# Joining the block inverses of a delta-rule layer to 64x64: two solves and one carry for each step in place of four and three

## The reference, cut to what matters

```
k_n = k / (norm(k) + 1e-6)
for t in range(768):
    y[t]  = q[t] @ state
    state = state + beta[t] * outer(k_n[t], v[t] - k_n[t] @ state)
```

## Time and profile before

| | us |
|---|---|
| median of three runs | 834.78 |
| profiled execution, its own time | 835.71 |
| its span | 834.0 |
| PE busy | 793.1 (95%) |
| DVE busy | 569.0 (68%) |
| ACT busy | 369.1 (44%) |
| POOL busy | 112.6 (14%) |

### The profile page before, as it was taken

One profiled execution on the slowest core, in us unless ns is written; L12 is line 12 of the kernel. 1 busy time (PEld: TensorE's weight loads), 2 busy tenths in 40 slices (PEclk: granted clock), 3 DMA queues, 4 the chain that ended last, 5 costly groups with the idle time before them and its releaser, 6 DMA issues.

```text
span 834.0 us, 29247 instructions
## 1 busy us (share of the span) xinstructions
PE 793.1 (95%) x12158; PEld 724.2 (87%) x12159; DVE 569.0 (68%) x1504; ACT 369.1 (44%) x1042; POOL 112.6 (14%) x281
## 2 busy tenths in 40 slices
PE   5978999999999999999999999999999989999994
PEld 3557888899989999889999999999999989999993
DVE  6967887878578685777777677654323667767751
ACT  3722443434435353443434535343543556666641
POOL 1000000001010010101002010000103054344441
PEclk9989999999999999999999999999999999999998
DMA  8743112121211223112220211211023546655610
GB/s 271 219 160 123 46 53 66 60 89 48 92 48 40 91 65 97 42 50 87 66 91 22 66 47 66 64 41 47 32 86 118 186 133 208 198 191 184 188 32 14
DMA packets 46649, 79.75 MB, mean 96 GB/s; under 512 B 5680, under 2 KB 35082, under 8 KB 46144
## 3 DMA queue, kind: packets, MB, share of 16 engines
q1 hardware_dynamic: 43104, 73.07, 27.1%
q0 software_dynamic: 3424, 4.93, 1.9%
HBM read 67.05 MB, written 13.19 MB: 96 GB/s over the span
## 4 chain that ended last, share of the span: by engine, by line
issue 79%; POOL 9%; DMA 6%; POOLq 2%; PE 2%; DVE 1%; ACT 0%; SPq 0%
DMA id_table<-token,slot 5%; POOL idle L680 3%; POOL kq_t L735 2%; POOL id_table L725 2%; PE psum L980 1%; POOL ids_all L731 1%; DMA id_table<-x_sb 1%; POOL out L790 1%; DMA kd<-kq 1%; POOLq L509 0%; POOLq L510 0%; PE psum L836 0%; POOLq L757 0%; POOL token L718 0%; PE psum L981 0%
## 5 line engine op out<-in xcount | busy, mean ns | idle before, releaser
L1014 PE MATMUL psum<-xt_hi,w_hi 128*128 128x256 f32 x768 | 226.3, 295 | 5.3 <-issue 2.7
L1015 PE MATMUL psum<-xt_lo,w_hi 128*128 128x256 f32 x768 | 217.5, 283 | 0.0
L1016 PE MATMUL psum<-xt_hi,w_lo 128*128 128x256 f32 x768 | 217.2, 283 | 0.0
L1190 ACT ACTIVATE h_raw<-psum 128x256 f32<-128x256 f32 x192 | 73.6, 384 | 311.0 <-PE psum L1016 309.3
L1449 DVE TENSOR_TENSOR h_lo<-h_raw,h_hi 128x256 fp32r<-128x256 f32 x192 | 81.4, 424 | 160.2 <-ACT h_hi L1191 159.4
L1014 PEld LDWEIGHTS psum<-xt_hi,w_hi 128*128 128x128 f32 x768 | 145.3, 189 | 14.5 <-issue 8.8
L1016 PEld LDWEIGHTS psum<-xt_hi,w_lo 128*128 128x128 f32 x768 | 146.3, 190 | 0.0
L1015 PEld LDWEIGHTS psum<-xt_lo,w_hi 128*128 128x128 f32 x768 | 145.8, 190 | 0.0
L1038 PE MATMUL psum<-w_hi,h_hi 128*128 128x394 f32 x384 | 138.6, 361 | 1.1 <-DVE h_lo L1449 1.1
L1040 PE MATMUL psum<-w_hi,h_lo 128*128 128x394 f32 x384 | 131.2, 342 | 0.0
L1039 PE MATMUL psum<-w_lo,h_hi 128*128 128x394 f32 x384 | 131.0, 341 | 0.0
(11 more groups left out here) (183 smaller groups left out, 1121.8 us busy)
## 6 DMA issues: line engine op xcount, KB each, us to landing
kq_t<-kq SPq DMA_DIRECT2D x24, 512.0 KB, 3.6
bp<-moe_w SPq DMA_DIRECT2D x24, 512.0 KB, 4.5
kv_t<-kv SPq DMA_DIRECT2D x24, 384.0 KB, 3.1
bp<-moe_w SPq DMA_DIRECT2D x24, 384.0 KB, 4.2
kd<-kq SPq DMA_DIRECT2D x20, 256.0 KB, 3.3
x_table<-x_sb SPq DMA_DIRECT2D x13, 392.0 KB, 2.8
out<-x_sb SPq DMA_DIRECT2D x12, 384.0 KB, 3.1
bp<-moe_w_in SPq DMA_DIRECT2D x6, 512.0 KB, 6.0
```

The costliest lines, as they stand in the source:

```text
L1014: m(out, hi, x_hi, start=first, stop=False)
L1015: m(out, hi, x_lo, start=False, stop=False)
L1016: return m(out, lo, x_hi, start=False, stop=last)
L1190: a_.activation(h_raw[i % 2][:, :], up_ps[i % 2][:, 0:G2], ACT.Silu)
```

## The change

**Joining inverses.** After the 32x32 inverses of a quad are ready, they are transposed a second time (`turn_first`, DVE). For each head and each pair of neighbouring blocks (0,1) and (2,3), PE multiplies the key block between them with the first block's inverse (`met`, 16 products of 32x32 by 32 columns for a step), ACT copies the result (`keep_met`), PE multiplies it with the second inverse (`grow`, 16 more), and DVE puts the product beside the two inverses (`grow`, two operations on 128 x 128 elements for a step), where ACT has spread them (`halves`, two copies of 128 x 512 for a pair). The result, `grown`, holds the inverses of 64x64 blocks. It lies in the old tiles `inv` and `dg`.

**The chain.** A step now has solve 0, carry, solve 1. A solve takes 8 products of 64x64 by 48 columns. The carry takes, for each a in 0, 1, first two products of 64 rows by 64 columns and then four of 64 rows by 32. ACT copies a solved half with two operations of 64 x 192 for a step, in place of four of 32 x 96 for each of four blocks.

**The order.** The chain of pair p begins at slot `BEGIN[p]` (9, 7, 5, 3, 1 slots into the period for p = 1 to 5, then 0), `halves` and `met` stand four slots ahead of it. The chain of pair 0 takes 12 slots instead of 27. Both halves of a `gram` stand in one slot, and the `diag` products stand in slots that hold other small products. `gram` uses banks 4 to 7 (`GRAM_BANK`). In the preamble `gram(1)` moves ahead of `rows(0)`, the 12 `warm` products go, and `turn_first`, `halves`, `met` and `grow` of pair 0 come in.

**The mixing of blocks.** `MIX = (0, 2, 1, 3)` takes the place of the head pair's number, so that two of four head pairs begin with the other half.

```diff
+        MIX = (0, 2, 1, 3)
+        x_odd = sb("x_odd", [P, Q // 2, Q])
+        parity = sb("parity", [P, 2])
+        grown = [... for x in (inv, dg)]
+        met_sb = [rest_sb[u][:, 0:H * Q]... for u in range(2)]
-        GRAM_BANK = {(0, 1): 6, (1, 0): 2, (1, 1): 6, (2, 0): 2, (2, 1): 2, (3, 0): 2}
+        GRAM_BANK = {(1, 0): 2, (2, 0): 2, (2, 1): 2}
-            return psum[:, GRAM_BANK.get((t, s), 4) + a, 2 * C * i:2 * C * i + 2 * C]
+            return psum[:, GRAM_BANK.get((t, s), 4 + 2 * s) + a, 2 * C * i:2 * C * i + 2 * C]
-        ROWS_AT = {4: 1, 13: 2}
-        SCORES_AT = {16: 0, 19: 1, 22: 2, 27: 3}
+        ROWS_AT = {2: 2}
+        SCORES_AT = {7: 0, 8: 1, 9: 2, 10: 3}
-        CHAIN = {0: ("read", 0), 3: ("solve", 0), 6: ("carry", 1), 9: ("solve", 1), 12: ("carry", 2), 15: ("solve", 2),
-                 18: ("carry", 3), 21: ("solve", 3), 24: ("update", 0), 26: ("keep", 0)}
+        BEGIN = {p: SLOTS * p + {1: 9, 2: 7, 3: 5, 4: 3, 5: 1}.get(p, 0) for p in range(1, NP + 1)}
+        CHAIN = {-4: ("halves", "met"), 0: ("grow", "read"), 3: ("solve0",), 6: ("carry",), 9: ("solve1", "queries"), 12: ("update", "outputs"), 14: ("keep",)}
+        FIRST_CHAIN = {0: ("solve0",), 3: ("carry",), 6: ("solve1", "queries"), 9: ("update", "outputs"), 11: ("keep",)}
+        for y, n, a in ((1, 2, 0), (10, 2, 1), (13, 3, 0), (SLOTS + 2, 3, 1)):
+            put(y, "gram", n, a)
+        for y, n, a in ((4, 2, 0), (12, 2, 1), (SLOTS + 1, 3, 0), (SLOTS + 3, 3, 1)):
+            put(y, "mask", n, a)
+        put(SLOTS, "scales", 2)
+        put(SLOTS + 5, "scales", 3)
+        for p in range(1, NP):
+            y, g = BEGIN[p], p // 2 + 1
+            for x, names in CHAIN.items():
+                put_pair(y + x, p, names)
+            if p % 2 == 0 and g < NQ:
+                for i, x in enumerate((-4, 6)):
+                    for n in range(2):
+                        put(y + x, "diag", g, 2 * i + n)
+                    for e in range(2):
+                        put(y + x + 1, "evict", g, i, e)
+            if p + 1 < NP:
+                for n in (2, 3):
+                    for a in range(2):
+                        put(y + 7 + 5 * n, "gram", 2 * p + n, a)
+                        put(y + 7 + 5 * n + 2 * a, "mask", 2 * p + n, a)
+                    put(min(y + 21 + 2 * n, SLOTS * p + SLOTS + n), "scales", 2 * p + n)
+        PREPARE = {11: ("squares", 0), 12: ("squares", 1), 13: ("turn",), 14: ("norms", 0), 15: ("norms", 1), 17: ("norms", 2), 19: ("spread",)}
+        FIRST_PREPARE = {7: ("squares", 0), 8: ("squares", 1), 14: ("turn",), SLOTS: ("norms", 0), SLOTS + 2: ("norms", 1),
+                         SLOTS + 4: ("norms", 2), SLOTS + 6: ("spread",)}
+            end = BEGIN[2 * g + 2] - 10
+            lane_at = lane_slots(range((BEGIN[2 * g] if g else 20) + 20, end))
+            put(end + 1, "turn_back", g + 1)
+            put(end + 2, "turn_first", g + 1)
...
             s["turn_back"](0)
-            for a in range(2):
-                s["mask"](1, a)
+            s["turn_first"](0)
+            s["halves"](0)
+            s["met"](0)
+            s["mask"](1, 0)
+            s["grow"](0)
+            s["rows"](1)
+            s["mask"](1, 1)
+            s["met"](1)
+            s["grow"](1)
...
+            def met(t):
...
+                pe.wait_ge(x_turned, g + 1)
+                pe.wait_ge(bp_ready, H * (t + 1) if t < 2 else H * (t // 2 * 2 + 2))
+                for h in HEADS:
+                    for n, first, second in odd_blocks(h):
+                        last = m(met_ps(t)[second, h, :], bp[t % NB][first, h, C:2 * C][:, key_block(n + 1)],
+                                 x_first[t // 2 % 2][first, H * (t % 2) + h, :], start=True, stop=True)
+            def grow(t):
...
+                for h in HEADS:
+                    for n, first, second in odd_blocks(h):
+                        last = m(grown_ps[u][first, h, :], met_sb[u][second, h, :], xt_blk[second, lane(t, h), :], start=True, stop=True)
+            def half_rows(h, b):
+                n = b ^ (MIX[h // 2] // 2)
+                return slice(2 * Q * n, 2 * Q * n + 2 * Q)
             def solve(t, b):
...
+                        rows = half_rows(h, b)
+                        last = m(s_ps[u][rows, head_cols(h)], grown_of(t)[rows, h, :], given[rows, head_cols(h)],
+                                 start=True, stop=True)
+            def carry(t):
...
+                for a in range(2):
+                    for hp in (2, 3, 0, 1):
+                        h = 2 * hp + a
+                        seen_by = half_rows(h, 0)
+                        keys = bp[t % NB][seen_by, h, C:2 * C]
+                        given = u_sb[u][seen_by, head_cols(h)]
+                        if hp >= HP // 2:
+                            last = m(r_ps[u][half_rows(h, 1), head_cols(h)], keys[:, 0:2 * Q], given, ...)
+                        else:
+                            for c in (2, 3):
+                                last = m(r_ps[u][block_rows(h, c), head_cols(h)], keys[:, key_block(c)], given, ...)
...
+            def turn_first(g):
+                d.transpose(low[:, :, :].rearrange("p b c -> p c b"), inv[:, :, :].rearrange("p i c -> p c i")).then_inc(x_turned, 1)
+            def grow(t):
...
+                for w in range(2):
+                    heads = slice(H // 2 * w, H // 2 * w + H // 2)
+                    beside = grown_of(t)[:, heads, Q * (1 - w):Q * (2 - w)]
+                    last = d.scalar_tensor_tensor(beside, grown_ps[t % 2][:, heads, :], minus_parity[:, w:w + 1], beside, ALU.mult, ALU.add)
```

More of the change, by code:

```diff
@@ L501, in steps @@
         def steps(**given):
-            names = [name for name, _ in CHAIN.values()]
-            names += ["mask", "diag", "evict", "squares", "norms", "spread", "scales", "gram", "turn", "lanes", "turn_back", "weights", "up", "lo", "down",
-                      "queries", "outputs", "rows", "scores", "first", "split", "x2", "choose", "rank", "place", "warm"]
+            names = [name for group in CHAIN.values() for name in group]
+            names += ["turn_first", "mask", "diag", "evict", "squares", "norms", "spread", "scales", "gram", "turn", "lanes", "turn_back", "weights", "up", "lo", "down",
+                      "rows", "scores", "first", "split", "x2", "choose", "rank", "place", "warm"]
             assert set(given) <= set(names)
@@ L879, in r_free, with read @@
                     after(pe, slot_ready, t // 2 - 2)
-            def read(t, b):
+            def read(t):
                 u = t % 2
```

298 lines of the change are left out of this document (163 added, 135 removed).

## The result

The changed kernel takes **897.69 us** (median of four runs, 895.05 to 900.26) against 835.06 for the kernel before beside it: 7.5% slower, ratio 1.075 with a 95% interval of 1.0715 to 1.0785. I had forecast 836.9 and a range to 845. The profiled execution is one of 895.05 us with a span of 893.4.

A forecast was written before the change was run, and what follows sets the result against it. PE's full queue was taken to bound the kernel from 135.85 to 640 us. 835.71 - 1.9 (periods 0 and 1) + 4.0 (steady stage) gave 837.8 profiled, 836.9 for the median; range for 8 in 10 828 to 845.

The forecast's parts named there:

- shorter waits between solves are worth nothing: Steady stage, 135.85 to 640 us: PE busy 501.63 of 504.15 us, so only number and form of its products count.
- mostly diag products waiting: Steady stage: PE's waits of 2.5 us in all; -2 counted for these waits and fewer diag insertions together.
- The work added on ACT [...] and DVE [...] I price at nothing from pair 2 on: Steady stage: `halves`, the `met` copy, second transposition and `grow` cost nothing, as each handover has three slots.
- +3 if that cover fails: Steady stage: if the three slots per handover don't suffice, say 0.3 us of waiting at a chain step in each pair.
- Double grams need `keep` done three slots earlier; that too is inside this cover: Steady stage: the earlier `keep` for merged grams fits the slack of three slots per handover, at no cost.
- +0.6 a pair: Steady stage: PE's sum of solves, carries, `met`, `grow` and edges for two steps; ten pairs +6 us.
- the third rival: 64x64 products run alone: solves +1.2 a pair, 849; half of it, 0.056 a start, 841. Chance 0.18 together with new waits.
- Period 0: 60 to 86 us: first solve at 63.8, first product of the next layer at 79.4 instead of 86.03, -6.6 us.
- Period 1: 86 to 135.85 us: PE waits 6.1 us for DVE, `met` from 90.6, slot 64 at 134.2; -1.9 left there.
- The carry doesn't drain: Rival: form changes in the carry cost no 0.14, carry 0.86, total 827.5; chance 0.32 together with period 0's gain staying.
- Products alone: Rival: two 64x64 pieces don't overlap, both solves cost 1.44, +12, 849; chance 0.18 together with new waits.
- New waits: Case of new waits, given no time of its own; chance 0.18 together with 64x64 products running alone.

The follow-up runs named there:

- run 11: Kernel of run 4 with the carry in 64x32 pieces alone: 862.4 us, ratio 1.034 to the kernel before.
- run 4: Changed kernel with ScalarE's copy `x_odd` ten slots later and VectorE's preparation of the next quad spread over other slots: 859.7 us, ratio 1.027.
- run 9: Changed kernel with ScalarE's copy later and VectorE's preparation spread in the even period only: 877.6 us, ratio 1.050.
- run 10: Changed kernel with ScalarE's copy later and VectorE's work spread only at the end before the next even period: 878.9 us, ratio 1.051.
- run 7: Kernel before, with one idle VectorE transposition a quad added in two halves in a crowded slot: 841.2 us, ratio 1.0054.
- run 2: Changed kernel with the carry's 64x64 products cut so that the whole carry is in 64x32 pieces: 896.1 us, ratio 1.071.
- third kernel: Changed kernel with ScalarE's copy `x_odd` ten slots later and the carry in 64x32 pieces only: 889.7 us, ratio 1.064.
- run 13: Kernel of run 11 with the two diag blocks of a slot put into neighbouring slots: 855.1 us, ratio 1.022.
- run 14: Kernel of run 11 with key products and masks moved by up to two slots, and the diag blocks in neighbouring slots: 845.9 us, ratio 1.011.

## Why the prediction was wrong

**Where the kernel was bound: right, and read too far.** PE's queue was full, and I concluded that "shorter waits between solves are worth nothing". That is true of the change's gain. I carried it over to the change's cost, where it doesn't hold. I also took the 2.5 us that PE did wait for "mostly diag products waiting". 1.1 of them were; 1.0 was `down` waiting for `lo`, in this line of the waits of the kernel before (137 to 640 us), so the `lo` was already the tight place:

```profile
PE psum L1038 <- DVE h_lo L1449: 1.0, 4, 0.2
```

**The step that failed: "The work added on ACT [...] and DVE [...] I price at nothing from pair 2 on: ACT was busy 20.35 of 48.20 and DVE 36.45".** A busy share of 76% is an average over a period. `down` needs a `lo` every two slots. Two slots are about 2.2 us, `lo` itself 0.42, so about 1.7 us of other work fit between two of them, with about a slot of slack behind. The diff put, in two stretches of each quad, 4 to 8 us between two `lo`: four masks within eight slots (grams were merged in pairs), a second transposition of 2.0 right behind a mask and ahead of `scales`, and the norms among the masks of the even period. Of PE's 34.5 idle us 30.4 are waits at `down` and `met` for VectorE (3.1 are stops as in run 11), and the lower clock, 0.92 to 0.97 in five passes, comes with them; runs 4, 9 and 10 take most of it away by position alone, and run 7 makes a small one on the kernel before. In the even period ScalarE's `spread` has a share that no run separates. My "+3 if that cover fails" had the right kind of loss at a tenth of the size, and at the wrong place: I counted handovers in the chain, each with three slots, and never `lo`, which has one. The rows were there: 1.95 for a transposition, 1.6 for four masks.

**"Double grams need `keep` done three slots earlier; that too is inside this cover".** The grams had no trouble. What they brought is that their masks come in bursts, which I didn't list among what a moved step issues.

**The price of the products: +0.6 a pair was +1.5.** The carry was right (1.84 forecast, 1.87 measured), and so was its reason, the change of form. A solve block is 1.07 and not 0.86, 0.42 a pair: with 0.14 for the form, two 64x64 starts take 0.058 and not 0.045, which is the half-way case that I had named in the third rival (0.056). `met` and `grow` are 0.76 and 0.75, not 0.69 each. The other 0.3 or so is in edges, of which I took 0.8 off. Alone this would have given 9 us more than my 836.9, about 846, at the edge of my range.

**Period 0: nearly right.** First solve 63.51 (63.8 forecast), carry 68.92 (69), first product of the next layer 80.78 (79.4), so -5.3 for -6.6.

**Period 1: right up to `met`, wrong behind it.** PE waited 5.0 us for VectorE (6.1 forecast), 2.19 and 2.73 of it at one time, and `met` started at 91.33 (90.6). But slot 64, forecast for 134.2 against 135.85 before, came at 137.03: a loss of 1.2 us and no gain of 1.9. From `met` on the period took 2.1 us more than my sum, with dearer products and a granted clock of 0.97. (The first product of the next pass also stands at 137.03, 1.2 us ahead of the 138.26 of before; but there a read and a diag block, 2.1 us, stand in front of it, which the changed kernel does later.) Up to `met` I did add up VectorE's instructions in their order, and it was the only place where I did; the same sum for one period of the steady stage would have shown the loss.

**Rivals.** "The carry doesn't drain" is refuted by run 2. "Products alone" was half true. "New waits" held, inside a case of 0.18 priced at 849. My sentence "I am wrong altogether if PE is no longer full from 136 us on" is what happened.

## What to carry over

When work is added to an engine that is not the bound, don't divide its busy time by the period. Find the step on it that the bound engine needs most often, take the interval between two of these less its own length, and lay every instruction that the change moves or adds into those gaps in queue order; what doesn't fit, beyond the slack behind, is mostly paid, and where it is paid moves with the slack. Do the same for a third engine that stands in its own order for one of the moved steps. Merging steps of the bound engine also merges what hangs on them elsewhere: masks here, and rows of short products in which PE stops. And where a cheaper step brings no time, list the waits by releaser before you say what took it: here it was not the engine that was waited for before.

## What the hardware showed that was not expected

- Changing between 64x64 and 64x32 products cost about 0.14 us each time (an estimate, 0.13 to 0.15): a carry with seven such changes inside took 1.87 us for 48 products, with none 0.81 for 64.
- Two 64x64 products of 48 columns start in about 0.058 us (32 in 1.07, less 0.14 for the form), against 0.045 for two of L953.
- PE stopped for up to 3.6 us (3.56 in the third kernel) at fixed counts of its instructions, with no releaser, and went on 1.1 to 1.7 us after a packet of 16 KB of its instruction queue had landed. The stops are long where rows of 128 to 192 short products stand; cutting the rows in two gave 7.2 and 6.1 us.
- Waits cost more than their length. The granted clock was 0.92 and 0.94 in two windows of the changed kernel with waits of 4.31 and 3.67 us, 0.50 right behind one of 3.91, and 1.00 over 503 us in the kernels with the waits mostly gone (runs 4, 13 and 14).
